# A three-part fused kernel: the second layer's output product in Strassen form

## The reference

```python
h = x @ w_in                                   # layer 1
P = a[0] + a[1] * h + a[2] * h2 + a[3] * h3
Q = 1.0 + np.abs(b[0]) * np.abs(h) + np.abs(b[1]) * h2
g = P / (Q + 1e-06)
x = g @ w_out
h = x @ w_in                                   # layer 2
sp = log1p(exp(min(h, 20)))                    # h itself above 20
g = h * np.tanh(sp)
return g @ w_out
```

## Time and profile before

| | us |
|---|---|
| median of 3 runs | 470.06 (469.83 to 472.02) |
| the profiled execution: its time | 470.82 |
| the profiled execution: its span, first to last instruction | 469.0 |
| mean granted TensorE clock | 0.995 of full |

### The profile page before, as it was taken

The page is one execution under the profiler, slowest core; times in us unless marked ns, Lnnn a source line. Parts: engine busy times, 40 slices in busy tenths (PEclk is TensorE's granted clock), DMA queues, the critical chain, the costliest instruction groups (busy, mean ns, idle before and its releaser), DMA issues.

```text
span 469.0 us, 10932 instructions
## 1 busy us (share of the span) xinstructions
PE 454.7 (97%) x4312; PEld 332.8 (71%) x4312; DVE 388.4 (83%) x658; ACT 306.2 (65%) x565; POOL 210.0 (45%) x228
## 2 busy tenths in 40 slices
PE   6997999999999999999999999999999999999997
PEld 5776878887888889899999975444445555557663
DVE  5777799999769787676879988889999888878894
ACT  4568798988657784778777777654745555554543
POOL 3878549874625313111227547258652222212122
PEclk9999899999999999999999999999999999999999
DMA  7998647323123000020011411112100200000101
GB/s 134 168 283 247 145 95 195 93 66 74 34 63 80 1 3 3 1 91 1 3 46 25 157 46 50 41 46 95 40 1 0 92 0 2 0 1 1 67 3 45
DMA packets 46544, 29.80 MB, mean 64 GB/s; under 512 B 31900, under 2 KB 40092, under 8 KB 46492
## 3 DMA queue, kind: packets, MB, share of 16 engines
q1 hardware_dynamic: 44972, 28.57, 23.1%
q10 hardware_dynamic: 1520, 0.53, 0.5%
HBM read 26.73 MB, written 2.36 MB: 62 GB/s over the span
## 4 chain that ended last, share of the span: by engine, by line
PE 86%; POOL 6%; DMA 3%; ACT 2%; SPq 1%; issue 1%; DVE 0%; ACTq 0%; POOLq 0%
PE bank L629 38%; PE bank L673 20%; PE bank L653 19%; PE bank L592 3%; DMA work<-in_moe_w_out 2%; POOL w L1103 1%; DMA late<-in_v 1%; PE bank L497 1%; POOL work L1101 1%; POOL g_l L1115 1%; PE bank L515 1%; PE bank L578 1%; POOL late L1103 1%; PE bank L533 1%; POOL late L1067 1%
## 5 line engine op out<-in xcount | busy, mean ns | idle before, releaser
L1115 POOL TENSOR_TENSOR g_l<-work,g_h 128x512 f16<-128x512 f32 (+2 forms) x81 | 88.4, 1092 | 224.2 <-ACT g_h L804 203.3
L629 PE MATMUL bank<-x_h,w 128*128 128x256 f16 (+1 forms) x640 | 102.3, 264 | 1.7 <-DVE x_l L941 1.6
L653 PE MATMUL bank<-g_h,w 128*128 128x256 f16 (+1 forms) x640 | 101.3, 262 | 0.6 <-POOL g_l L1115 0.6
L629 PE MATMUL bank<-x_h,late 128*128 128x512 f16 (+2 forms) x384 | 96.9, 326 | 0.0
L794 ACT ACTIVATE bank<-work,coef 128x512 f32<-128x512 f32 (+2 forms) x81 | 52.4, 647 | 66.9 <-DVE work L971 64.0
L673 PE MATMUL bank<-late,g_h 128*128 128x512 f16 x288 | 92.0, 379 | 0.0
L629 PE MATMUL bank<-x_l,w 128*128 128x256 f16 (+1 forms) x320 | 84.4, 264 | 0.0
L653 PE MATMUL bank<-g_l,w 128*128 128x256 f16 (+1 forms) x320 | 83.8, 262 | 0.0
L653 PEld LDWEIGHTS bank<-g_h,w 128*128 128x128 f16 x640 | 60.9, 98 | 8.6 <-issue 2.8
L629 PEld LDWEIGHTS bank<-x_h,w 128*128 128x128 f16 x640 | 61.3, 98 | 7.5 <-issue 1.9
L629 PE MATMUL bank<-x_l,late 128*128 128x512 f16 (+2 forms) x192 | 62.6, 326 | 0.0
(11 more groups left out here) (103 smaller groups left out, 776.9 us busy)
## 6 DMA issues: line engine op xcount, KB each, us to landing
raw<-in_moe_w_in SPq DMA_DIRECT2D x10, 512.0 KB, 4.5
raw<-in_moe_w_out SPq DMA_DIRECT2D x10, 512.0 KB, 4.0
late<-in_k SPq DMA_DIRECT2D x16, 144.0 KB, 3.9
late<-in_v SPq DMA_DIRECT2D x8, 288.0 KB
late<-in_moe_w_out SPq DMA_DIRECT2D x4, 512.0 KB, 4.3
late<-in_moe_w_in SPq DMA_DIRECT2D x4, 512.0 KB, 4.1
out<-w SPq DMA_DIRECT2D x8, 256.0 KB, 2.5
late<-in_v SPq DMA_DIRECT2D x15, 97.5 KB
```

What stands on the lines that cost most here:

```text
L629: last = pe.matmul(ps, w_in(l, wp)[:, kk, at], x[:, kk, t0:t0 + n], start=(kk == 0 and wp == 0 and x is x_h), stop=(kk == KD - 1 and wp == 1))
L653: last = pe.matmul(ps, w_out(0, wp)[:, f, 128 * d:128 * (d + 1)], g[q % 4][:, i * n:(i + 1) * n], start=False, stop=(f == FT - 1 and d % 2 ...
L1115: pool.tensor_tensor(g_l[q % 4][:, 0:w], num[q % 4][:, 0:w], g_h[q % 4][:, 0:w], ALU.subtract).then_inc(g_rest, 1)
```

## The change

Layer 2's output product takes blocks of 256 tokens (`BLOCKS2` = four of 256, one of 128) and, for each pair of groups of 128 hidden columns, forms the product of 2 x 2 blocks (token halves x hidden halves of g; hidden halves x column halves of w_out, 256 columns each) by the Winograd variant of Strassen's scheme: seven block products in place of eight. Seven accumulators of 128 x 256 take three and a half banks. The last block of 128 tokens multiplies in the plain way.

- GpSimd makes the sums of weights in float32 (`fold`, eight of them), ScalarE their heads (1024 and 768 wide, after the fold), GpSimd their rests (1024 and 768 wide). Folds 4 to 7 are kept where layer 1's w_in was.
- GpSimd also makes the sums of g (`add_up`, one 256-wide and two 128-wide steps); ScalarE writes two heads, GpSimd two rests (384 and 512 wide) for each of the 32 paired tiles.
- The factor e + 2 is written to the PSUM bank of the reciprocal by ScalarE (`factor`), VectorE multiplies it from there; the last product is ordered so that t r is formed in the same bank first.
- VectorE adds the seven products up while they leave PSUM (`leave_y2`).
- The table of ticks of units 16 to 31 is another one, and eight folds stand in it.

```diff
-    BLOCKS2 = [(0, 512), (512, 384), (896, 256)]
+    BLOCKS2 = [(0, 256), (256, 256), (512, 256), (768, 256), (1024, 128)]
+    PRODUCTS = [(0, 0, 0, 0), (2, 2, 0, 1), (5, 5, 1, 0), (3, 1, 1, 1), (4, 4, 2, 0), (6, 3, 2, 1), (1, 6, 3, 0)]
+              ("pool", "fold", (98.5, 102.5, 106.5, 110.5, 114.5, 124.5, 132.5, 139.5))]
-             (16, 85.4, 103.05, 123.625, 1),
-             (17, 192.562, 96.875, 119.0, 1),
...
-             (31, 234.425, 165.475, 166.875, 1)]
+             (16, 127.14, 100.3, 101.3, 0),
+             (17, 127.145, 100, 101, 1),
+             (18, 127.147, 104.3, 105.3, 0),
+             (19, 127.15, 104, 105, 1),
+             (20, 127.212, 108.3, 109.3, 0),
+             (21, 127.215, 108, 109, 1),
+             (22, 127.252, 112.3, 113.3, 0),
+             (23, 127.255, 112, 113, 1),
+             (24, 127.292, 116.3, 117.3, 0),
+             (25, 127.295, 120, 122, 1),
+             (26, 127.332, 120.3, 121.3, 0),
+             (27, 127.335, 128, 130, 1),
+             (28, 127.372, 124.3, 125.3, 0),
+             (29, 127.425, 135.2, 137.2, 1),
+             (30, 127.412, 128.3, 129.3, 0),
+             (31, 127.505, 142.2, 144.2, 1)]
...  output_second
+                    for i, (gi, wi, bank, half) in enumerate(PRODUCTS if paired else single):
+                        elif first:
+                            pe.wait_ge(y2_left, 4 * (b - 1) + bank + 1)
+                            if begin and whole:
+                                pe.matmul(y2_bank[bank][:, :], g, beside_zeros(wi), start=True, stop=False)
+                            else:
+                                last = pe.matmul(y2_bank[bank][:, HW * half:HW * (half + 1)], g,
+                                                 folded(j, wp)[:, HW * wi:HW * (wi + 1)], start=begin,
...  ScalarE: weight_head, factor, head_sums, the loop
+                if is_folded(u):
+                    act.wait_ge(w_folded, 6 * (j + 1))
+                    if j >= 4:
+                        act.wait_ge(h_ready, N1 - FT // 2 + 2 * (j - 4) + 2)
+                    act.activation(folded(j, 0)[:, 0:2 * DM], stage[slot], ACT.Copy)
+                    act.activation(folded(j, 0)[:, 2 * DM:FOLDS * HW], w_sums, ACT.Copy).then_inc(w_head, 1)
+                act.activation(inv_bank[q % 2][:, 0:w], ab[q % 2][:, 0:w], ACT.Identity, bias=two).then_inc(factor_done, 1)
+                act.activation(g_h[q % 4][:, :], sums[q % 2], ACT.Copy).then_inc(g_head, 1)
                 if m < NT:
                     estimate(m)
+                if m - 2 in PAIRED:
+                    head_sums(m - 2)
...  VectorE: fraction, quotient, leave_y2
-                        dve.scalar_tensor_tensor(out=d, in0=d, scalar=2.0, in1=d, op0=ALU.add,
+                        dve.scalar_tensor_tensor(out=d, in0=inv_bank[q % 2][:, 0:w], scalar=EXP_20 + 2.0, in1=d, op0=ALU.min,
+                    dve.tensor_tensor(r, t, r, ALU.mult).then_inc(nr_done, 1)
-                        dve.tensor_tensor(t, t, d, ALU.mult).then_inc(g_done, 1)
+                    dve.scalar_tensor_tensor(out=t, in0=d, scalar=2.0 * K2, in1=r, op0=ALU.subtract,
+                                             op1=ALU.mult).then_inc(g_done, 1)
+                c21, c22, c11, c12 = [rows[:, DM * row + HW * i:DM * row + HW * (i + 1)] for i in range(4)]
+                add(c11, p[1], c21).then_inc(y2_left, 1)
+                add(c22, p[2], c21).then_inc(y2_sum, 1)
...
+                add(c21, p[6], c21).then_inc(y2_left, 1)
...  GpSimd: fold, weight_rest, add_up, rest
+                    pool.tensor_scalar(x[:, half], x[:, half], WS, 1.0, ALU.mult, ALU.mult).then_inc(w_folded, 1)
+                pool.tensor_tensor(t1, b12, b11, ALU.subtract).then_inc(w_folded, 1)
+                pool.tensor_tensor(b12, b12, b22, ALU.add).then_inc(w_folded, 1)
+                pool.tensor_tensor(t2, b22, t1, ALU.add).then_inc(w_folded, 1)
+                pool.tensor_tensor(t4, b21, t2, ALU.subtract).then_inc(w_folded, 1)
+                if q in PAIRED:
+                    add_up(q)
+                    pool.wait_ge(g_head, g_parts(q) - 1)
+                    pool.tensor_tensor(g_wide[1][q % 4], num[q % 4][:, 128:w], g_wide[0][q % 4], ALU.subtract).then_inc(g_rest, 1)
+                    pool.wait_ge(g_head, g_parts(q))
+                    pool.tensor_tensor(g_l[q % 4][:, :], sums[q % 2], g_h[q % 4][:, :], ALU.subtract).then_inc(g_rest, 1)
```

More of the change, by code:

```diff
@@ L77, in attention_moe_moe @@
     ROWS = B * S // 128
+    PAIRED = [q for q, (l, _, _, n, _, _) in enumerate(tiles) if l == 1 and n == 256]
+    HW = DM // 2
+    FOLDS = 7
+    PRODUCTS = [(0, 0, 0, 0), (2, 2, 0, 1), (5, 5, 1, 0), (3, 1, 1, 1), (4, 4, 2, 0), (6, 3, 2, 1), (1, 6, 3, 0)]
     LAYERS, PREFILL, SLOT = 39.125, 4.25, 2.5
@@ L215, in w_in, with w_out, folded, beside_zeros @@
         def w_in(l, part):
[L216 to L222, removed]
+            return layers[l][:, 0:2 * WH].rearrange("p (u w k f) -> p u w k f", u=FT // 2, w=2, k=KD)[:, :, part, :, :]
+        def w_out(part):
+            return w1[:, (2 + part) * WH:(3 + part) * WH].rearrange("p (f d) -> p f d", f=FT)
+        def folded(j, part):
+            home, at = (w2, 2 * WH + 2 * FOLDS * HW * j) if j < 4 else (w1, 4 * KD * 256 * (j - 4))
+            at += FOLDS * HW * part + (HW if j < 4 and (j > 0 or part == 1) else 0)
+            return home[:, at:at + FOLDS * HW]
+        no_weight = w2[:, 2 * WH + FOLDS * HW:2 * WH + (FOLDS + 1) * HW]
+        def beside_zeros(wi):
+            at, apart = 2 * WH + HW * wi, HW * (FOLDS - wi)
+            return w2[:, at:at + 2 * apart].rearrange("p (i n) -> p i n", i=2)[:, :, 0:HW]
+        rows = w1[:, 2 * WH:2 * WH + 2 * ROWS * DM].bitcast(F32)
         carved = [0]
@@ L263, in attention_moe_moe, with g_piece @@
                  + [late[:, LATE + 1024 * i:LATE + 1024 * (i + 1)] for i in range(2)])
-        g_h = [sb(f"g_h{i}", [128, WIDE], F16) for i in range(4)]
-        g_l = [sb(f"g_l{i}", [128, WIDE], F16) for i in range(4)]
+        end = late[:, LATE + 2048:LATE + TAIL]
+        g_own = [[sb(f"g_{x}{i}", [128, WIDE], F16) for i in range(4)] for x in "hl"]
+        g_wide = [[end[:, 192 * (4 * x + i):192 * (4 * x + i + 1)].bitcast(F16) for i in range(4)] for x in range(2)]
+        sums = [end[:, 1536 + 512 * i:2048 + 512 * i] for i in range(2)]
+        w_sums = raw[:, 0, 0:3 * HW]
+        g_h, g_l = g_own
+        def g_piece(x, q, i):
+            return g_own[x][q % 4][:, 128 * (i - 3):128 * (i - 2)] if i >= 3 else g_wide[x][q % 4][:, 128 * i:128 * (i + 1)]
         masks = sb("masks", [128, 2 * (UG + 3), KW], BF16)
@@ L389, in unit, with is_folded, g_parts @@
             if u % 2 == 0:
-                return w_in(l, part)[:, :, f * 128:(f + 2) * 128]
-            return w_out(l, part)[:, f:f + 2, :]
+                return w_in(l, part)[:, f // 2, :, :]
+            return w_out(part)[:, f:f + 2, :]
+        def is_folded(u):
+            return u >= FT and u % 2 == 1
+        def g_parts(q):
+            return q + 1 + sum(p <= q for p in PAIRED)
         def staged(u):
@@ L660, in output_second @@
                 _, b, t0, n, many, f0 = tiles[q]
[L661 to L677, removed]
+                pe.wait_ge(g_rest, g_parts(q))
@@ L772, in first_reads @@
                 act.wait_ge(h_ready, q + 1)
-                if q >= 3:
+                if q >= 3 and layer == 0:
                     act.wait_ge(g_done, q - 2)
@@ L791, in estimate @@
                 act.wait_ge(den_done, q + 1)
-                if q >= 2:
+                if q >= 2 and layer == 0:
                     act.wait_ge(nr_done, q - 1)
@@ L1013, in leave_y @@
                 else:
[L1014 to L1021 removed]
+                    leave_y2(b)
             dve.memset(k_all[0:64, :, 1, :], 0.0).then_inc(zeroed, 1)
```

194 lines of the change are left out of this document (137 added, 57 removed).

## The result

The changed kernel takes 534.2 us in the median (530.4 to 535.8) where the kernel before takes 470.1 in the same comparison: ratio 1.134, 95% interval 1.127 to 1.141. The profiled execution has a span of 531.2 us, 62.2 more than before.

A forecast was written before the change was run, and what follows sets the result against it. TensorE, busy 97% of a 469.0 us span, was taken as the bound. Terms -6.9 + 31 + 1 + 3 + 13 + 6 = +47 on the profiled 470.82 gave 518, a median of 517 us, range 480 to 538.

The forecast's parts named there:

- Term 2: Folding weights, slots 24 to 30: GpSimd and ScalarE take turns, making low parts late, +31 us (+14 to +38).
- Terms 3 and 4: Later folds and units delay GpSimd's rests, +1 us (0 to 4); head 31 and unit 31 at step 42, +3 (0 to 6).
- Term 1: TensorE's own second-layer work falls from 186.8 to 179.9 us, -6.9; -2.1 with the skill's 81 ns at 128 columns.
- Term 5: Second layer: head of sums behind the estimate makes L 5.7 us and slots 5.3, +13 us over 32 tiles (0 to 25).
- Term 6: Ends of blocks: VectorE's seven additions from PSUM delay the next step, 4 times 1.5, +6 us (0 to 8).
- rival D: Clock falls from 2.4 to 1.2 GHz in long waits, +4 us at slots behind, 521; within the forecast's range, 0.57 together.
- Rival A: GpSimd alone sets slots 24 to 30, heads fitting its shadow: 14 us in place of 31, 500 us; chance 0.18.
- Rival C: Faster: TensorE stays the bound, every rest ends before its slot, only the 6.9 us saving is seen, 463 us; chance 0.09.

The follow-up runs named there:

- narrow: unscaled with GpSimd's folding instructions about an eighth as wide and the rests' part of the product reading the heads: 468.5 us, ratio 0.988 to the kernel before.
- sums_early: The changed kernel with one ScalarE reordering: head of the sums of tile m-2 ahead of the estimate of tile m: 516.3 us, ratio 1.093 to the kernel before.
- quotient: The kernel before with only layer 2's quotient through PSUM: 471.9 us, ratio 0.999.
- whole: split with the pieces of each fold and folded rest together again, heads still behind their folds: 509.7 us, ratio 1.075 to the kernel before.
- split: The changed kernel with folds and folded rests in three pieces, heads in two, each behind its fold: 498.9 us, ratio 1.060 to the kernel before.
- unscaled: split plus the early head of sums, folded weights not scaled by 256, pieces moved to end before slot 41: 486.5 us, ratio 1.025 to the kernel before.

## Why the prediction was right, step by step

I forecast 517 us, range 480 to 538; 534.2 came, 17 above and near the upper end. The mechanism was right, the sizes of the waits too small. In the profile 62.2 us came for 47: 4.6 by chance at the start, 6.2 more than term 2, 7.6 more than terms 3 and 4, and 3.3 less than terms 1, 5 and 6 together.

- **Term 1, TensorE's work, -6.9.** Right: 109 and 56 ns, and narrow's second layer gains 5.0 after some 2 at the ends of blocks (its three ends take 0.6 to 0.7 each). The 81 ns at 128 columns of the Trainium skill (page "TensorE: Matmul & The Clock Gate", section "Back-to-back issue gap") does not hold here: 56 measured, with a weight load for each.
- **Term 2, folds up to slot 30, +31.** Measured 35.7 up to the start of slot 30, 37.2 up to slot 31. Slots 24 to 30 were late by 4.7, 7.2, 3.1, 5.6, 2.9, 6.9, 5.2 us where I had 4.5, 4.6, 2.6, 6.1, 0.8, 7.2, 5.2. The order of the queues gave this pattern, with one place misread: head 19 has tick 104 and the head of step 27 has 35.875 + 2.5 x 27.3 = 104.125, so tile 25's head stood behind head 19 and its wait for fold 1. GpSimd had finished the fold at 237.99 and got tile 25's head only at 240.37 (the lines of L1231, L829 and L883 above): 2.4 us of slot 25's 7.2. The other excess is in durations. VectorE's rest of an even unit took 3.17 us once, in place of 1.2 (the seven others 1.2 to 1.5), while GpSimd worked on a folded rest, and stood ahead of half a step; fold 4 took 5.94 in place of 4.4, its two scalings 2.50. And TensorE's clock fell, my rival D: slot 28 was late by 2.9 mostly because the two products of slot 27 took 6.9 us for 3.96. TensorE's waits in slots 24 to 30 are 25.2 us, and the rest of the 37.2, 12.0 us, is its products taking longer; but between 219 and 284.9 no product stands in the chain that ended last, so most of these 12.0 lay where TensorE would have waited. In the chain the clock shows in slot 30's output product, 1.6 us (3.61 for 1.98).
- **Terms 3 and 4, later items, +1 and +3.** The step that failed most: 8.7 measured before slot 40. Behind it the first eight slots take 45.8 us where eight steady ones take 42.9; 1.6 of these 2.9 is slot 40's output product, 4.24 us for 2.63 at 0.61 of the full clock. I had let a fold cost 4.4 us and counted the head start of 1.6 us anew for each. In the chain a fold here and the low part behind it:

```profile
298.66 2.15 POOL raw L1224 x2
...
301.61 1.00 POOL raw L1227
302.61 1.00 POOL raw L1229
...
304.38 0.90 POOL g_l L1278
```

Two scalings take 2.15 us (1.66 reckoned) and two of its steps 1.00 each (0.67). VectorE's steps with two SBUF inputs beside them take 0.90 and 1.08 for 0.60. Behind one whole item the head start is gone when the next comes. The longest wait, 3.9 us at slot 40, is a turn again: fold 7 ends at 334.17, ScalarE's head 31 comes after it, and the head of the sums that slot 40 needs (337.31) stands behind head 31 and the estimate.
- **Term 5, the chain head of sums to low part, +13.** L = 5.7 reckoned, 5.6 in the steady slots, slots 5.36 for 5.3; moving the one instruction gave back 13.3 us. Shown by experiment.
- **Term 6, the ends of blocks, +6.** Three slots at an end take 6.53, 4.92 and 5.70, 1.1 us over three steady ones: 3.3 for the three ends between blocks of 256, less than I took (the fourth falls in the last block). Without the long chain (sums_early) an end costs 0.6 to 0.7.
- **Not in the sum:** 4.6 us at the start, which the stretches above show to be chance: quotient, which has the attention stage of the kernel before, shows 4.1 and the same mean clock of 0.85 in its first 70 us, and sums_early, which has the change's, shows 0.7 at 0.98. Without it the total would lie in my range too.

Rival A, GpSimd's amount of work alone: whole and split have the same amount and lose 20.5 and 16.3 us where the change loses 45.9, so the amount alone does not make 45.9. It is not nothing either: the 16.3 go when the folding is left out (narrow). Rival C, TensorE stays the bound, came true only in narrow, where the folding is left out. No division of the folding between the engines that hides it was found, and none is excluded; the best placement tried is 10 us above the kernel before.

## What to carry to other kernels

An operation moved to an engine that is idle half of the time must still fit between two of the instructions that another engine waits for; cut it in pieces shorter than that gap, and place its consumer where the wait has surely ended, for a wait in an in-order queue holds up everything behind it, and two engines that wait for each other in turn lose the sum of their work. In a software pipeline look at the latency from a stage's input to what the matrix engine needs, not only at each engine's sum: a new instruction belongs ahead of the long wait in its queue. Before saving one eighth of a product, subtract what narrower instructions give back and ask what else the saved time has to pay for.

## What the runs showed of the hardware that I had not expected

- A VectorE instruction with two SBUF inputs of 1024 columns took 3.17 us in the change and 2.17 in unscaled beside GpSimd, 1.2 alone; GpSimd's low part doubled (1.89 for 0.91) in the same place. Both sides pay.
- In the change three of VectorE's steps of 384 columns with two SBUF inputs took 1.68, 1.69 and 1.99 us for 0.60 beside a folded rest on GpSimd, and each ended 0.4 us behind the end of the GpSimd instruction that it met (at 232.05, 260.45 and 262.37 us), as if it had waited for that end. If so, what VectorE loses depends on the length of GpSimd's instruction; no run varies that length alone.
- Matmuls of 128 columns with a weight load for each ran at 56 ns: the 53.3 ns of 128 columns at 2.4 GHz, and 2.7 more.
- The granted clock averaged 0.80 over the 60 us (220 to 280) in which TensorE's waits were 4.6, 5.5, 5.5 and 4.9 us, with 6 to 11 us of work between them; in split, with waits of at most 1.2 us there, it was 1.00.
